# A long convolution by four transform stages and two MLPs on one core: each half's fourth stage follows its third, and the spectral product is stored channel by channel

## The chip, the cores and the metric

One core of a Trainium2 chip (trn2) runs the whole program. The metric is the device time of one execution in microseconds.

## The reference

For 12480 positions and 128 channels, `x` and `v` are given. A small network makes a filter of the same length for each channel, `h = relu(pos_emb @ w1) @ w2`, times a decay over positions. Then

```python
u = x * v
Uf, Hf = rfft(u, n=2 * S), rfft(h_filt, n=2 * S)
y = irfft(Uf * Hf, n=2 * S)[:S]
x1 = x * y
x2 = square(relu(x1 @ moe_w_in)) @ moe_w_out
g = x2 @ moe2_w_in
out = (g * sigmoid(1.702 * g)) @ moe2_w_out
```

with a hidden width of 2048 in both MLPs. All inputs are float32.

## The kernel before

Positions are an array of A = 104 rows by B = 120 columns. The transform of twice that length is four rounds of matrix products with constant tables.

- The filter network comes first (lines 703 to 724).
- Stage 1 (`step1`, line 731) transforms over the 104 rows, for 64 channels (a half, `h`) of the filter H and then of u. Its results are copied to Z, 124 partitions.
- Stage 2 (`step2`, line 780) transforms over the columns in NG = 26 groups of four frequencies. A group is 4 products of 256 columns. ACT copies the filter's half of the spectrum from PSUM (`copy_h`, line 604), VectorE multiplies (`products`, lines 663 to 673) into `prod_s` and `prod_x`, and GpSimd combines these into the real and imaginary product P with one subtraction and one addition (`combine_p`, lines 332 to 337; `combine`, line 519). Group 25 is combined by VectorE (line 679). `prod_s` and `prod_x` have two buffers each. P is laid out [120 partitions][frequency 104][real, imaginary][channel 64].
- Stage 3 (`step3`, line 745) transforms back over the columns, in 16 groups of four channels. P is the stationary operand, `P[h][:, :, r, 4 * k + e]`, 104 columns with a step of 128 elements. ACT copies two edges and the imaginary part (lines 615 to 624), and VectorE makes a difference and a sum of it for Y (lines 681 to 689), iterating channel, real/imaginary, column.
- Stage 4 (`step4`, line 397) transforms back over the rows and brings both halves' channels to positions. It comes once, after both halves' stages 1 to 3: 15 groups plus a single column group, each with both halves, with tables in a ring `t4` of four. 12 groups and the single column are done before the MLPs, 3 groups (LATE) inside the first MLP tile at positions 2, 4 and 6 of its order (`LATE_AT`). ACT and VectorE copy 64 partitions at a time to XT (lines 379 to 395), GpSimd multiplies x and y to a tile (`stage`, line 917).
- The MLPs (`mlps`, line 816) run over 30 tiles of 416 positions, each product as three products of rounded parts (lines 1005 to 1010). Weights are loaded raw, rounded by ACT (`make_hi`) and split by GpSimd (`split_low`, two operations for each of four weights).

So the halves run 1, 2, 3, 1, 2, 3, 4, MLP. Stages share four PSUM slots of two banks; a slot's user waits on `free[q]`. SP's queue issues nearly all loads in the order written out at lines 444 to 492 and waits in that order. In stage 2 it refills a ring of four spectrum table buffers `f_ring` (240 KB each) as TensorE leaves them. Ahead of that in the first half it issues `load_u(1, 0)` and `load_u(1, 1)` (four loads of 390 KB); in the second half, four t4 tables (338 KB each) and the last column's. `load_u(1, i)` brings x and v of 8 channels, which GpSimd multiplies and folds (`make_u`, lines 495 to 505, one product and two sums); for the second half this starts right behind the first half's combinations. Small products on constants (`spare_products`) fill TensorE's waits between stages.

Of the kernel before, what the change touches and what calls it, by code (L numbers as in the profile page):

```python
# [5 lines left out]
S = 12480  # L6
A, B = 104, 120
L = 2 * S
# [27 lines left out]
LATE = 3  # L36
EARLY = [*range(JG - LATE), JG]
LATE_AT = {2: JG - 3, 4: JG - 2, 6: JG - 1}
# [3 lines left out]
Y_HALF = B * D  # L42
HR = 2 * Y_HALF
BIG = HR + 2 * HC * BR
U_ZONE = HC * BR
U_SLACK = 3 * 2 * FG * 2 * HC


def constant_tables(w1, w2):
# [14 lines left out]
    t4.append(2 * np.pi * np.outer(f + 0.5, (a - A // 2) * B + B) / L)  # L64
# [16 lines left out]
def s4_units(g):  # L81

    return g + 1 + (g >= JG - LATE)


def tile_rows(t):

    g = t // 2
    if t % 2 == 0:
        return [TB * g + i for i in range(TB)]  # L90
    if g == JG - 1:
        return [B - 1, *range(B - 1 - LOW + 1, B - 1 - LOW + TB)]
    return [B - 1 - TB * (g + 1) + i for i in range(TB)]


TILE_ORDER = [b for t in range(NT) for b in tile_rows(t)]
# [8 lines left out]
def by_tile(z):  # L105

    return z.reshape(A, B, D)[:, TILE_ORDER].transpose(2, 1, 0).reshape(D, S)


def from_tiles(z):  # L110

    out = np.empty((A, B, D), z.dtype)
    out[:, TILE_ORDER] = z.reshape(D, B, A).transpose(2, 1, 0)
    return out.reshape(S, D)


def build(nc, x_ch, v_ch, x_t, pos_emb, w_in1, w_out1, w_in2, w_out2,
# [10 lines left out]
    with ExitStack() as ctx:  # L128
# [9 lines left out]
        with ExitStack() as shared:  # L138
            mlp = mlp_buffers(lambda name, shape, dt=F32: sb(name, shape, dt, shared), F32R)
        conv = conv_buffers(sb)  # L140
        XT = conv["big"][:, HR:HR + S].rearrange("p (t n) -> p t n", n=TN)

        first = {name: sem(name) for name in (
            "s4_full", "xt_low", "xt_high", "x_t_in0", "x_t_in1", "staged", "x1_hi", "x1_lo")}
        w_hi_made = [sem(f"w_hi_made{m}") for m in range(4)]
        w_split = [sem(f"w_split{m}") for m in range(4)]
        weights = (w_in1, w_out1, w_in2, w_out2), w_in_dma, mlp["w_hi"], mlp["w_lo"], w_hi_made, w_split

        block = ctx.enter_context(nc.Block())
        late = convolution(nc, block, sem, ALU, ACT, ds, F32, ps, conv, mlp, XT, weights, first,  # L150
                           x_ch, v_ch, x_t, pe_d, net, fwd1, fwd2_d, inv3, inv4, identity)
        mlps(nc, block, sem, ALU, ACT, ds, F32, XT, ps, mlp, weights, first, late, x_t, out)


def conv_buffers(sb):

    return {
        "big": sb("big", [128, BIG]),
        "u_zone": sb("u_zone", [128, U_ZONE]),
        "t3": sb("t3", [B, 184]),  # L160
        "t1": sb("t1", [A, 2, 2 * A]),
        "f_ring": sb("f_ring", [128, RING, FG, B]),
    }


def mlp_buffers(sb, F32R):
# [8 lines left out]
    def skip_to(where):  # L175
        assert where >= at[0], (where, at[0])
        if where > at[0]:
# [3 lines left out]
           "in_hi": [None] * 2, "in_lo": [None] * 2, "x_tile": [None] * 2}  # L181
    pair = [128, 2, TN]

    out["w_lo"][2] = put("w_lo2", [128, DFF], F32R)
    out["w_lo"][3] = put("w_lo3", [128, DFF], F32R)
    out["relu"] = put("relu", pair)
    out["act_f"] = [put(f"act_f{s}", pair) for s in range(NS)]
    out["act_hi"] = [put(f"act_hi{s}", pair, F32R) for s in range(4)]
    out["yT"] = put("yT", [128, TN])
    assert at[0] <= Y_HALF - LATE * TB * 2 * D  # L190
    skip_to(Y_HALF)
    out["w_hi"][2] = put("w_hi2", [128, DFF], F32R)
    out["w_hi"][3] = put("w_hi3", [128, DFF], F32R)
    out["act_hi"] += [put(f"act_hi{s}", pair, F32R) for s in range(4, NB)]
    out["act_lo"] = [put(f"act_lo{s}", pair, F32R) for s in range(NB)]
    out["in_hi"][1] = put("in_hi1", [128, TN], F32R)
    out["in_lo"][1] = put("in_lo1", [128, TN], F32R)
    assert at[0] <= 2 * Y_HALF - LATE * TB * 2 * D
    skip_to(HR + S)
    out["in_hi"][0] = put("in_hi0", [128, TN], F32R)  # L200
    out["in_lo"][0] = put("in_lo0", [128, TN], F32R)
    assert at[0] == HR + A * 2 * HC + 2 * TN - (A * 2 * HC - S)
    out["w_hi"][0] = put("w_hi0", [128, DFF], F32R)
    out["x_tile"][0] = put("x_tile0", [128, TN])
    skip_to(BIG)
    out["w_lo"][0] = put("w_lo0", [128, DFF], F32R)
    out["w_lo"][1] = put("w_lo1", [128, DFF], F32R)
    skip_to(BIG + U_ZONE - (RING * TB * TAB + TAB))
    out["t4"] = put("t4", [128, RING, TB, TAB])
# [880 lines left out]
```

## Time and profile before

| | us |
|---|---|
| median of 3 runs | 1504.84 (1504.59 to 1507.27) |
| the profiled execution | 1502.83 |
| its span | 1501.0 |
| TensorE busy in it | 1477.3 |
| ScalarE (ACT) busy | 999.2 |
| VectorE (DVE) busy | 914.5 |
| GpSimd (POOL) busy | 197.3 |

The profile is of one execution, and its durations are compared with its own time. PEld is the load of the stationary operand, which overlaps products. Products are pipelined, so the recorded duration of one is longer than the pace; the pace comes from a stage's time divided by its instructions. Of a product in full float32 the trace has two instructions.

### The profile page before, as it was taken

The numbers are of one execution on the slowest core, as the hardware profiler recorded it, in microseconds if no ns is written. First come the engines' busy times: TensorE is split into PE (matmuls) and PEld (weight loads), VectorE is DVE, ScalarE is ACT, GpSimd is POOL, SyncE is SP. The second block draws the span as 40 slices with busy tenths as digits, with TensorE's granted clock in tenths as the row PEclk, the third lists the DMA queues.
The fourth block names the chain that finished last, engine by engine and source line by source line (L and its number), as shares of the span: only waits on it lengthen the run. The fifth ranks groups of instructions, "written<-read, shape, count | busy, mean of one in ns | idle before, by whom it ended". The sixth has DMA issues, their size and how long they took to land.

```text
span 1501.0 us, 22451 instructions
## 1 busy us (share of the span) xinstructions
PE 1477.3 (98%) x7970; PEld 1434.4 (96%) x7970; DVE 914.5 (61%) x1198; ACT 999.2 (67%) x1404; POOL 197.3 (13%) x192
## 2 busy tenths in 40 slices
PE   8999999999999999999999999999999999999998
PEld 6987998899989999999999999999999999999997
DVE  3668576663556666666666666666666566666664
ACT  6643254323577777777777777777777777777775
POOL 5418802602300000000000000000000000000000
PEclk9999999999999999999999999999999999999999
DMA  8223503405100000000000000000000000000000
GB/s 224 74 78 110 154 1 93 124 1 158 46 1 12 12 11 11 11 11 11 11 11 11 11 12 19 15 11 11 11 11 11 11 11 11 12 11 11 6 6 12
DMA packets 28344, 52.06 MB, mean 35 GB/s; under 512 B 3060, under 2 KB 22140, under 8 KB 28052
## 3 DMA queue, kind: packets, MB, share of 16 engines
q1 hardware_dynamic: 27768, 51.02, 11.5%
q10 hardware_dynamic: 540, 0.55, 0.1%
q8 instruction: 23, 0.38, 0.1%
q14 instruction: 13, 0.11, 0.0%
HBM read 45.17 MB, written 6.39 MB: 34 GB/s over the span
## 4 chain that ended last, share of the span: by engine, by line
PE 96%; DVE 1%; DMA 1%; ACT 1%; issue 1%; SPq 0%; ACTq 0%
PE ps L1008 24%; PE ps L1010 24%; PE ps L1009 24%; PE ps L751 6%; PE ps L741 6%; PE ps L786 5%; PE ps L408 3%; PE ps L722 2%; DMA f_ring<-in_fwd 1%; PE ps L715 1%; DVE act_lo L996 1%; PE ps L707 0%; PE ps L729 0%; ACT act_f L951 0%; DVE act_hi L994 0%
## 5 line engine op out<-in xcount | busy, mean ns | idle before, releaser
L996 DVE TENSOR_TENSOR act_lo<-act_f,act_hi 128x832 fp32r<-128x832 f32 x480 | 489.1, 1029 | 126.8 <-ACT act_hi L954 118.5
L1008 PE MATMUL ps<-in_hi,w_hi 128*128 128x416 f32 x960 | 338.4, 353 | 6.4 <-DVE in_lo L968 2.6
L1008 PE MATMUL ps<-act_hi,w_hi 128*128 128x416 f32 x960 | 339.0, 353 | 0.9 <-DVE act_lo L996 0.9
L1009 PE MATMUL ps<-act_lo,w_hi 128*128 128x416 f32 x960 | 337.5, 352 | 0.0
L1010 PE MATMUL ps<-act_hi,w_lo 128*128 128x416 f32 x960 | 336.7, 351 | 0.0
L1010 PE MATMUL ps<-in_hi,w_lo 128*128 128x416 f32 x960 | 336.3, 350 | 0.0
L1009 PE MATMUL ps<-in_lo,w_hi 128*128 128x416 f32 x960 | 336.2, 350 | 0.0
L994 DVE CAST act_hi<-act_f 128x832 fp32r<-128x832 f32 x240 | 143.7, 599 | 296.9 <-ACT act_f L949 296.9
L944 ACT ACTIVATE relu<-ps 128x832 f32<-128x832 f32 x240 | 208.3, 868 | 131.7 <-PE ps L1010 127.4
L951 ACT ACTIVATE act_f<-ps 128x832 f32<-128x832 f32 x240 | 207.0, 862 | 107.5 <-PE ps L1010 107.3
L949 ACT ACTIVATE act_f<-relu 128x832 f32<-128x832 f32 x240 | 215.9, 900 | 22.1 <-DVE act_lo L996 0.4
L954 ACT ACTIVATE act_hi<-ps 128x832 fp32r<-128x832 f32 x240 | 206.0, 858 | 0.0
L1008 PEld LDWEIGHTS ps<-in_hi,w_hi 128*128 128x128 f32 x960 | 180.2, 188 | 10.0 <-issue 5.1
L1008 PEld LDWEIGHTS ps<-act_hi,w_hi 128*128 128x128 f32 x960 | 179.7, 187 | 3.9 <-DVE act_lo L996 2.0
L1010 PEld LDWEIGHTS ps<-act_hi,w_lo 128*128 128x128 f32 x960 | 180.9, 188 | 2.6
L1009 PEld LDWEIGHTS ps<-in_lo,w_hi 128*128 128x128 f32 x960 | 180.1, 188 | 2.6
L1010 PEld LDWEIGHTS ps<-in_hi,w_lo 128*128 128x128 f32 x960 | 180.3, 188 | 2.2
L1009 PEld LDWEIGHTS ps<-act_lo,w_hi 128*128 128x128 f32 x960 | 180.2, 188 | 1.7
L751 PEld LDWEIGHTS ps<-t,big 120*104 120x104 f32 x512 | 91.9, 273 | 4.2 <-issue 4.2
L751 PE MATMUL ps<-t,big 120*104 120x120 f32 x512 | 92.2, 344 | 3.7 <-issue 3.7
L786 PE MATMUL ps<-big,f_ring 124*120 (+1 forms) x416 | 90.7, 380 | 4.0 <-DMA f_ring<-in_fwd 3.4
L786 PEld LDWEIGHTS ps<-big,f_ring 124*120 124x120 f32 x416 | 75.8, 183 | 18.7 <-issue 4.2
(79 smaller groups left out, 1118.9 us busy)
## 6 DMA issues: line engine op xcount, KB each, us to landing
f_ring<-in_fwd SPq DMA_DIRECT2D x52, 240.0 KB, 2.6
big<-in_x_by_channel SPq DMA_DIRECT2D x16, 390.0 KB
big<-in_v_by_channel SPq DMA_DIRECT2D x16, 390.0 KB
out<-yT SPq DMA_DIRECT2D x30, 208.0 KB, 1.9
t<-in_inv SPq DMA_DIRECT2D x15, 338.0 KB
big<-in_pos_emb SPq DMA_DIRECT2D x40, 78.0 KB
x_tile<-in_x_by_tile SPq DMA_DIRECT2D x15, 208.0 KB, 2.6
t<-in_x_by_tile SPq DMA_DIRECT2D x15, 208.0 KB, 2.5
```

The lines of the kernel that those rows point to most:

```text
L741: mm = nc.tensor.matmul(slot[q][0:BR, e // 2, at:at + 2 * A], data, t1[:, 1 if k < N1 // 2 else 0, :], start=True, stop=True)
L751: mm = nc.tensor.matmul(slot[q][0:A, e // 2, at:at + W3], P[h][:, :, r, 4 * k + e], t3[:, r * (LOW + 1):r * (LOW + 1) + W3], start=True, s ...
L786: mm = nc.tensor.matmul(flat[s][0:B, j * 2 * D:(j + 1) * 2 * D], f_ring[0:BR, s, j, :], Z[h][:, :, ds((k * FG + j) * 2 * HC, 2 * HC)], sta ...
L944: nc.scalar.activation(relu[:, :, :], slot[s], ACT.Relu).then_inc(relu_done, 1)
L949: nc.scalar.activation(act_f[s][:, :, :], relu[:, :, :], ACT.Square).then_inc(act_done[0], 1)
L951: nc.scalar.activation(act_f[s][:, :, :], slot[s], ACT.Gelu_apprx_sigmoid)
L954: nc.scalar.activation(act_hi[p % NB][:, :, :], slot[s], ACT.Gelu_apprx_sigmoid)\
L994: nc.vector.tensor_copy(hi[:, :, :], f[:, :, :]).then_inc(hi_done, 1)
L996: nc.vector.tensor_tensor(lo[:, :, :], f[:, :, :], hi[:, :, :].bitcast(F32), ALU.subtract)\
L1008: nc.tensor.matmul(to, w_hi[w][:, cols], hi, start=first, stop=False)
L1009: nc.tensor.matmul(to, w_hi[w][:, cols], lo, start=False, stop=False)
L1010: return nc.tensor.matmul(to, w_lo[w][:, cols], hi, start=False, stop=last)
```

## The change

It does three things.

1. The fourth stage of a half follows its third: 1, 2, 3, 4, 1, 2, 3, 4, MLP. A group now has one half in one bank, 128 partitions by 416 positions, and ACT alone copies it (`keep_xy`) to X[h]. The first half has 15 groups, the second 10 ahead of the MLPs and 5 (LATE) inside the first tile, at positions 2, 4, 6, 16 and 17, copied by VectorE. Each half's t4 tables are loaded. The two halves' rows are brought together by DMAs (`load_xy`) into `xy_tile`, from which GpSimd multiplies.
2. Memory is laid out anew, and loads move in SP's queue with it. In the first half, no load of x and v is issued ahead of stage 2's tables; all eight pieces come after the combination. In both halves the first four refills of `f_ring` are ahead of what follows. GpSimd waits for VectorE's last combination before it folds.
3. P is laid out [120 partitions][channel 64][real, imaginary][frequency 104]. The combination iterates channel and then frequency, and VectorE's third-stage operations iterate column and then channel.

```diff
-LATE = 3
-LATE_AT = {2: JG - 3, 4: JG - 2, 6: JG - 1}
+LATE = 5
+LATE_AT = {2: JG - 5, 4: JG - 4, 6: JG - 3, 16: JG - 2, 17: JG - 1}
...
-    P = [carve(big, B, (h + 1) * Y_HALF, A, 2, HC)[0] for h in range(2)]
+    P = [carve(big, B, at, HC, 2, A)[0] for at in P_AT]
...
         rows = ds(k * FG, FG)
-        s, x = prod_s[h][:, half], prod_x[h][:, half]
-        tensor_tensor(P[h][:, rows, 0, :], s[:, :, 0, :], s[:, :, 1, :], ALU.subtract)
-        tensor_tensor(P[h][:, rows, 1, :], x[:, :, 0, :], x[:, :, 1, :], ALU.add).then_inc(p_done[half], 1)
+        to = P[h][:, :, :, rows].rearrange("p c r f -> p r c f")
+        s, x = (prod[h][:, half].rearrange("p f r c -> p r c f") for prod in (prod_s, prod_x))
+        tensor_tensor(to[:, 0], s[:, 0], s[:, 1], ALU.subtract)
+        tensor_tensor(to[:, 1], x[:, 0], x[:, 1], ALU.add).then_inc(p_done[half], 1)
...
-                    mm = nc.tensor.matmul(slot[q][0:A, e // 2, at:at + W3], P[h][:, :, r, 4 * k + e],
+                    mm = nc.tensor.matmul(slot[q][0:A, e // 2, at:at + W3], P[h][:, 4 * k + e, r, :],
...
-                low, high = (Y[h][:, 0:LOW - 1, :, m, c4].rearrange("p j r c -> p c r j") for m in (h, 1 - h))
-                re2 = re.rearrange("p c (r j) -> p c r j", r=2)[:, :, :, 1:LOW]
-                im2 = im_copy[h][:, k % 2].rearrange("p c (r j) -> p c r j", r=2)[:, :, :, 0:LOW - 1]
+                low, high = (Y[h][:, 0:LOW - 1, :, m, c4].rearrange("p j r c -> p r j c") for m in (h, 1 - h))
+                re2 = re.rearrange("p c (r j) -> p r j c", r=2)[:, :, 1:LOW, :]
+                im2 = im_copy[h][:, k % 2].rearrange("p c (r j) -> p r j c", r=2)[:, :, 0:LOW - 1, :]
...
+    def keep_xy(copy, h, g, q):
+
+        to, made, last = X[h][:, g], ps[:, 2 * q, 0:TN], ps[:, 2 * q + 1, TN - A:TN]
+        if g < JG - 1:
+            return copy(to, made)
...
+    def load_xy(sp, t):
+
+        n, g = t % 2, t // 2
+        sp.dma_start(mlp["x_tile"][n][:, :], x_t[:, t * TN:(t + 1) * TN]).then_inc(x_t_in[n], 16)
+        for h in range(2):
+            rows = slice((t + h) % 2 * HC, ((t + h) % 2 + 1) * HC)
+            sp.dma_start(mlp["xy_tile"][n][h * HC:(h + 1) * HC, :], X[h][rows, g]).then_inc(x_t_in[n], 16)
...
         for h in range(2):
-            if h == 0:
-
-                stage_done(sp, "s1", 0)
-                load_u(1, 0)
-                load_u(1, 1)
-            else:
+            for s in range(RING):
+                load_f(h, 1, s)
+            if h == 1:
 
                 stage_done(sp, "s1", 1)
                 for g in range(RING):
-                    load_t4(g)
-                sp.dma_start(t4_last[0:A, :], inv4[:, JG * TB * TAB:]).then_inc(t4_last_in, 16)
-            with sp.Fori(1, F_FULL) as i:
+                    load_t4(sp, 1, g)
+                sp.dma_start(t4_last[1], inv4[:, JG * TB * TAB:]).then_inc(t4_last_in, 16)
+            with sp.Fori(2, F_FULL) as i:
...
             if h == 0:
+                for g in range(RING):
+                    load_t4(sp, 0, g)
+                for i in range(PIECES):
+                    if i >= X_SLOTS:
+
+                        sp.wait_ge(u_folded, PIECES + i - X_SLOTS + 1)
+                    load_u(1, i)
+                    if i == X_SLOTS - 1:
+                        sp.dma_start(t4_last[0], inv4[:, JG * TB * TAB:]).then_inc(t4_last_in, 16)
+                load_t4_behind(0, range(RING, JG))
+
+                stage_done(sp, "s4", 0)
                 for s in range(RING):
                     sp.dma_start(f_ring[:, s], fwd2_d[:, s * FG:(s + 1) * FG, :]).then_inc(ld_f[s], 16)
...
+        for m in range(3):
+            load_w(m)
+        stage_done(sp, "s3", 1)
+        load_w(3)
+        load_t4_behind(1, range(RING, RING + 2))
+
+        s4_done(sp, 0)
+        sp.wait_ge(free[0], used["s4", 1][0] + 1)
+        load_xy(sp, 0)
+        load_t4_behind(1, range(RING + 2, JG - 1))
...
             if h == 0:
+
+                p_made(pool, 0)
+                stage_done(pool, "s2", 0)
+                nc.gpsimd.memset(U[1][:, :, LOW:ODD], 0.0)
                 for i in range(PIECES):
                     make_u(1, i)
...
+            for k, spare in ((N3 - 4, 1), (N3 - 3, 2), (N3 - 2, 2)):
+                q = k % RING
+                pe.wait_ge(free[q], used["s3", h][q] + k // RING + 1)
+                spare_products(q, spare)
+            y_made(pe, h)
+            for g in range(JG - h * LATE):
+                q = g % RING
+                pe.wait_ge(free[q], used["s4", h][q] + g // RING)
+                step4(pe, h, g, q, full[q])
```

`load_t4_behind` waits for TensorE to leave a group's table buffer before it loads the next into it. ACT rounds the four weights at groups 0, 2, 5 and 8 of the second half's fourth stage.

## Rows read from the trace of the kernel before

**Rows 1.** The profile's part 1: busy time (share of the span) and instructions of each engine.
```profile
PE 1477.3 (98%) x7970; PEld 1434.4 (96%) x7970; DVE 914.5 (61%) x1198; ACT 999.2 (67%) x1404; POOL 197.3 (13%) x192
```

**Rows 2.** Busy time by stage: window, its length, then PE, PEld, DVE, ACT, POOL busy (x instructions), clock, DMA.
```profile
98.10:145.20 47.10, 45.25 (x209) 38.09 (x210) 33.42 (x75) 14.63 (x25) 33.62 (x48) 1.00 0.53 148
...
150.99:197.08 46.09, 46.09 (x256) 46.09 (x257) 26.71 (x30) 10.39 (x45) 33.01 (x22) 0.97 0.41 126
342.20:386.19 43.99, 43.99 (x392) 43.81 (x392) 14.39 (x25) 16.18 (x27) 14.81 (x7) 1.00 0.55 159
```

**Rows 3.** Groups by line and form, TensorE's loads: busy us, mean ns, idle before.
```profile
L751 PEld LDWEIGHTS ps<-t,big 120*104 120x104 f32 x512 | 91.9, 273 | 4.2 <-issue 4.2
L786 PEld LDWEIGHTS ps<-big,f_ring 124*120 124x120 f32 x416 | 75.8, 183 | 18.7 <-issue 4.2 <-DVE big L318 1.1
L408 PEld LDWEIGHTS ps<-t,big 104*128 104x128 f32 x480 | 54.1, 192 | 1.6 <-issue 1.5
...
L722 PEld LDWEIGHTS ps<-big 128*104 128x104 f32 x120 | 21.1, 176 | 7.5 <-ACT big L557 0.3 <-issue 0.2
```

**Rows 4.** TensorE in order of time: start us, us, what, idle before it.
```profile
107.09 38.24 PE L786 MATMUL ps<-big,f_ring 124*120 x176 [1.84 <-DMA f_ring<-in_fwd]
...
150.99 46.26 PE L751 MATMUL ps<-t,big 120*104 120x120 f32 x256 [3.21 <-issue]
...
243.58 7.14 PE L786 MATMUL ps<-big,f_ring 124*120 124x256 f32 x32 [0.29 <-DVE big L318]
252.28 38.22 PE L786 MATMUL ps<-big,f_ring 124*120 x176 [1.56 <-DMA f_ring<-in_fwd]
...
293.40 45.98 PE L751 MATMUL ps<-t,big 120*104 120x120 f32 x256 [0.46 <-issue]
...
342.20 43.10 PE L408 MATMUL ps<-t,big 104*128 104x104 f32 x384 [1.29 <-DVE big L689]
```

**Rows 5.** Groups by line and form, VectorE: third stage, products, first stage's copies.
```profile
L318 DVE COPY big<-ps 64x832 f32<-64x832 f32 x32 | 32.5, 1017 | 23.9 <-PE ps L741 23.9
...
L670 DVE TENSOR_TENSOR u_zone<-ps,u_zone 120x512 f32<-120x512 f32 x26 | 18.0, 691 | 14.0 <-ACT u_zone L609 14.0
...
L688 DVE TENSOR_TENSOR big<-ps,u_zone 104x472 f32<-104x472 f32 x16 | 15.4, 963 | 20.4 <-ACT u_zone L624 20.4
```

**Rows 6.** GpSimd in order of time, combinations of the second stage.
```profile
102.30 0.72 POOL L336 TENSOR_TENSOR big<-big 120x256 f32 x1 [47.88 <-DVE big L672]
...
142.36 0.73 POOL L336 TENSOR_TENSOR big<-big 120x256 f32 x1 [0.31 <-DVE big L672]
143.05 0.73 POOL L337 TENSOR_TENSOR big<-big 120x256 f32 x1
144.09 0.72 POOL L336 TENSOR_TENSOR big<-big 120x256 f32 x1 [0.31 <-DVE big L672]
```

**Rows 7.** Groups by line and form, GpSimd: product of x and v, fold, weight split.
```profile
L501 POOL TENSOR_TENSOR big<-big 104x960 f32<-104x960 f32 x16 | 35.7, 2229 | 19.2 <-DMA big<-in_v_by_channel 19.2
...
L503 POOL TENSOR_TENSOR u_zone<-big 104x480 f32<-104x480 f32 x16 | 19.3, 1208 | 1.3
...
L511 POOL TENSOR_TENSOR w_lo<-u_zone,w_hi 128x1024 fp32r<-128x1024 f32 x4 | 9.3, 2352 | 64.9 <-ACT w_hi L571 64.9
```

**Rows 8.** VectorE's last combination beside GpSimd's folding (order of time), and alone (groups).
```profile
147.07 2.20 POOL L501 TENSOR_TENSOR big<-big 104x960 f32<-104x960 f32 x1
...
147.37 2.18 DVE L336 TENSOR_TENSOR big<-big 120x256 f32<-120x256 f32 x1
...
L336 DVE TENSOR_TENSOR big<-u_zone 120x256 f32<-120x256 f32 x1 | 0.4, 424 | 0.0
```

**Rows 9.** The window after TensorE's longest idle time, columns as in rows 2.
```profile
151.00:152.00 1.00, 1.00 (x5) 1.00 (x6) 0.00 (x0) 0.00 (x0) 1.00 (x2) 0.50 0.08 13
```

**Rows 10.** SP's queue in order of time at the second half's tables, and the loads' sizes.
```profile
242.35 1.57 SPq L432 DMA_DIRECT2D t<-in_inv  x4
...
t<-in_inv SPq DMA_DIRECT2D x15, 338.0 KB
```

More of the change, by code:

```diff
@@ L163, in conv_buffers, with raw_weights @@
     }
+def raw_weights(sb):
+    w_raw, end = [None] * 4, 0
+    for m, at in ((3, X_SIZE + DFF), (0, Z_AT[1][0]), (1, Z_AT[1][0] + 2 * DFF), (2, Z_AT[1][0] + 4 * DFF + 3 * TN)):
+        sb(f"below_w_raw{m}", at - end)
+        w_raw[m] = sb(f"w_raw{m}", DFF)[:, :]
+        end = at + DFF
+    return w_raw
 def mlp_buffers(sb, F32R):
@@ L214, in mlp_buffers @@
-    out["x_tile"][1] = out["t4"][:, 3, 0:2, :].rearrange("p i w -> p (i w)")
+    out["stage"] = put("stage", [128, TN])
+    out["w_lo"][2] = put("w_lo2", [128, DFF], F32R)
+    for n in range(2):
+        out["x_tile"][n] = put(f"x_tile{n}", [128, TN])
+        out["xy_tile"][n] = put(f"xy_tile{n}", [128, TN])
+    skip_to(Y_AT[1])
+    out["act_hi"] = [put(f"act_hi{s}", pair, F32R) for s in range(NB)]
+    out["act_lo"] = [put(f"act_lo{s}", pair, F32R) for s in range(NB)]
+    assert at[0] <= Y_AT[1] + (JG - LATE) * TB * 2 * D
@@ L215, in mlp_buffers, with convolution @@
+    skip_to(Y_AT[1] + Y_SIZE)
+    out["relu"] = put("relu", pair)
+    out["yT"] = put("yT", [128, TN])
+    skip_to(IM_AT[1])
+    out["act_f"] = [put("act_f0", pair)]
+    skip_to(BIG)
+    out["act_f"] += [put(f"act_f{s}", pair) for s in range(1, NS)]
     return out
-def convolution(nc, block, sem, ALU, ACT, ds, F32, ps, buf, mlp, XT, weights, first,
+def convolution(nc, block, sem, ALU, ACT, ds, F32, ps, buf, mlp, X, weights, first,
                 x_ch, v_ch, x_t, pe_d, net, fwd1, fwd2_d, inv3, inv4, identity):
@@ L301, in convolution @@
     for h in range(2):
-        for name, groups in (("s1", N1), ("s2", NG), ("s3", N3)):
+        for name, groups in (("s1", N1), ("s2", NG), ("s3", N3), ("s4", JG - h * LATE)):
             used[name, h] = list(n)
@@ L308, in convolution @@
     P_USES = [len(range(s, NG, 2)) for s in range(2)]
+    T4_USES = [len(range(s, JG, RING)) for s in range(RING)]
     def step1_channels(k, h):
@@ L412, in _, with s4_done @@
+    def load_xy(sp, t):
[4 more added lines that the diff above has]
+            sp.dma_start(mlp["xy_tile"][n][h * HC:(h + 1) * HC, :], X[h][rows, g]).then_inc(x_t_in[n], 16)
+    def s4_done(eng, h):
+        for q in range(RING):
+            eng.wait_ge(free[q], used["s4 end", h][q])
     @block.sync
@@ L895, in _ @@
     def _(sp):
[L896 to L900 removed]
+        for q in range(RING):
+            banks_free(sp, q)
+        load_xy(sp, 1)
+        sp.wait_ge(s4_late, 1)
+        load_t4(sp, 1, JG - 1)
         sp.wait_ge(staged, 1)
[L902 removed]
+        load_xy(sp, 2)
         for r in range(NT):
@@ L1045, in part @@
                     if found is None:
-                        before = max(n for n in range(len(EARLY)) if n % RING == p % NS)
-                        pe.wait_ge(xt_low, min(before + 1, JG - LATE))
-                        pe.wait_ge(xt_high, before + 1)
+                        banks_free(pe, p % NS)
                     else:
```

305 lines of the change are left out of this document (126 added, 179 removed).

## The prediction

> **What bounds the kernel now.** I read the engine shares first, then the busy time by stage, then TensorE's loads by form, then the order of time where stages meet. TensorE is busy 98% of the span [rows 1], so only its speed in a stage, or its idle time between stages, can move the end. The stages of one half of the channels are: the second (208 TensorE instructions, with GpSimd at 33.62 of 47.10 us), the third (256 in 46.09 us) and the fourth (392 in 43.99 us, for both halves) [rows 2]. A product in full precision is recorded as two instructions, so the numbers per instruction below are halves of a product.
>
> The third stage stands out. Its 256 instructions take 46.26 us, 181 ns each, though each streams 120 columns only. The second stage streams 256 columns in 38.24/176 = 217 ns, 0.85 ns a column. The loads say why: a load of 104 columns takes 273 ns where the operand is read with a step of 512 bytes, and 176 to 192 ns where 104, 120 or 128 columns lie side by side [rows 3]. In the windows of rows 2, loading is busy for the whole of the third stage and for 38.09 of 47.10 us of the second.
>
> **The change part by part.**
>
> *The third stage.* With side-by-side columns the load no longer sets the pace. Streaming would be 120 x 0.85 = 102 ns; the fourth stage, 104 columns streamed and 128 loaded side by side, has 43.99/392 = 112 ns. I take 104 ns, bounds 102 and 112: 256 x 0.104 = 26.6 us for a half, against 46.26 and 45.98 us [rows 4]. VectorE must keep up: 16 groups of two operations, 963 ns each on the record. Today they read runs and write with a 1 KB step, where a 512-element operation with unstrided writes takes 691 ns, so the step costs about 0.6 ns an element; the new order writes runs of 16 bytes, as a copy of 832 elements in 1017 ns does at full pace, but its SBUF input gets a 480-byte step [rows 5]. Bounds 0.65 and 0.96 us for one, 1.3 to 1.9 us for a group against TensorE's 1.66; recorded operations overlap a little, so I take 1.69. Third stage: 27.0 us a half, together **-38.2 us**.
>
> *The combination on GpSimd.* This pays for it. Today each group has a pair of subtractions and additions of 120x256, 0.73 us each and 1.42 us together, and then 0.31 us of waiting: GpSimd has 18% to spare in a period of 1.73 us [rows 6]. Afterwards both inputs are read with a step of 512 bytes and the output is written in runs of four. No GpSimd row with such a step exists. From contiguous rows, 2229 ns for 960 elements and 1208 for 480, an operation is 0.19 us plus 2.13 ns an element [rows 7]. The lower bound is no change. For the middle I take the two strided prices of other engines: TensorE's load, (273-176)/104 = 0.9 ns a column [rows 3], and VectorE's 0.6 ns an element [rows 5]. Two inputs make 1.2 to 1.8 ns more, so one operation is 1.04 to 1.19 us, a pair 2.0 to 2.3. I take 2.15 us, as these are the nearest strided accesses. The upper bound is two strided accesses in turn at their whole recorded cost, VectorE's 963/472 = 2.0 ns or the load's 273/104 = 2.6 ns, 1.2 to 1.5 us for one operation.
>
> The Trainium skill's GPSIMD Engine Reference, "Performance pitfalls for Q7 kernels", says that a GpSimd kernel reading SBUF with a step over 8 bytes pays about 2.9 cycles an element instead of 1.9, half as much again. No row here shows it. By it on the whole element cost, one operation would be 1.0 us and the pair 1.95, five microseconds less per half than my term; if its extra cycle, at the page's 1.2 GHz, is paid for each input, the pair is 2.25.
>
> At 2.15 us GpSimd sets the pace of the second stage. Its first pair starts 4.2 us after the stage's first product (102.30 [rows 6], where the stage's window begins at 98.10 [rows 2]). 25 groups then take 53.8 us. The last group is combined by VectorE, which has two inputs in SBUF: beside a GpSimd operation this took 2178 ns, alone 424 [rows 8], so I add 1.0 us. The third stage then begins 59.0 us after the second. Today it is 150.99-98.10 = 52.9 us and 293.40-243.58 = 49.8 us [rows 4]. **+6.1 and +9.2 us**. In the first half this already includes the removal of two waits: 3.21 us before 150.99, since the new wait keeps GpSimd's folding off VectorE's last combination, and 1.84 us before 107.09, where the spectrum table stood behind four loads of x and v [rows 4, 8]. After those 3.21 us of idle time the granted clock was 0.50, 1.2 of 2.4 GHz, in the window from 151 us [rows 9]; today's load-bound products hardly feel that, streaming-bound ones would, and a slow GpSimd leaves a like wait. **+1.0 us** for both halves.
>
> *The fourth stage cut in two.* The same 488 instructions remain; 244 now run behind the first third stage, 160 before the MLP and 84 inside it. ACT alone copies them, one 128-row copy per group. In the old stage ACT and VectorE together were busy 30.6 of 43.99 us [rows 2], so that is hidden. What is new is a second passage from third to fourth: 293.40+45.98 = 339.38 to 342.20 [rows 4], **+2.8 us**.
>
> *Loads moved past each other.* All eight pieces of x and v for the second half now leave behind four t4 loads, and t4 group 4 leaves behind the eighth piece, which waits until five pieces are folded. A piece costs GpSimd 2.23+2x1.21 = 4.65 us [rows 7]. The first needs 1.4 MB of tables and 0.8 MB of its own: some 12 us, from the 1.68 MB that took 252.28-242.35 = 9.9 us [rows 4, 10]. So five pieces are done at 35 us behind the combination, and t4 group 4 lands about 6 to 7 us later, 42. TensorE wants it at 27.0+2.8+4x1.8 = 37. **+4 us**, bounds 0 and 6. The folding itself ends at 12+37 = 49 us, long before its reader. In the second half the t4 tables now leave after 4 spectrum loads, some 7.5 us into the stage. The same 9.9 us put the next spectrum table at 17.4, wanted at 8x1.73 = 13.9 with today's pace, 17.2 with GpSimd's: nothing beside 2.15 us, but 3.5 instead of 1.56 us if GpSimd is not the bound.
>
> *The MLP's start.* Weights have 18 us of fourth stage instead of 44, and GpSimd needs 2.35 us per split, eight of them [rows 7]. The first two and the first product of x and y fit; the last two end some 4 us into the first tile, as now, and are wanted two tiles later. Five late groups of the fourth stage are spread over the first tile instead of three double ones. The rest of the MLP keeps its instructions; the xy tiles come by DMAs that SP issues a tile ahead. 0, bounds -1.5 and +2.
>
> **Sum:** -38.2+15.3+1.0+2.8+4 = -15.1. The profiled execution took 1502.8 us; 1487.7 by its own time. It lies 2.0 us under the median of the runs, 1504.84, so I forecast 1489.
>
> **The rivals.**
>
> *GpSimd stays hidden* (pair at most 1.7 us). For it: it has 0.31 us to spare, and its 2.13 ns an element is slow enough to hide a slower fetch. Then the second stages take 52.9-1.84-2.75 = 48.3 and 49.8+1.9 = 51.7 us, -2.7 instead of +15.3; with -38.2+1+2.8+4 that is -33: **1472**, and 1468 without the t4 wait.
>
> *GpSimd takes away more than the third stage gives.* This one ends slower. Place: the same pairs. If GpSimd serves its two strided reads in turn, an operation is 1.4 us, between 1.2 and 1.5 of the upper bound, and the pair 2.8: 4.2+70+1 = 75 us per second stage, +22+25 = +47, -38+47+3 for the slow clock after longer idle+2.8+4 = +19: **1523**. It decides from where the second stages grow by 30 us together, a pair of 2.45 us. Against it: no strided row adds over 0.9 ns an element, and this needs 1.3 for each input.
>
> Read as 2.9 cycles for each input in turn, the Trainium skill's figure (the same page and section) would lead here.
>
> *The third stage doesn't speed up*, since VectorE's new order is slower than the old one, 1.3 us and more an operation, or since the load's 273 ns do not come from the step. Third stage 41 us a half gives only 10 back: 1500 with a hidden GpSimd, **1518** with a slow one. The side-by-side loads of rows 3 speak against the second reason.
>
> **How the numbers follow.** Forecast 0.43, hidden 0.30, GpSimd too slow 0.17, third stage not faster 0.06, something else 0.04, shared out. The range 1466 to 1512 takes in the first two with their bounds and the near part of the others; the forecast's own range is 1478 to 1502. A measurement can tell 0.2%, 3 us. Faster 0.78, same 0.03, slower 0.19.
>
> **What would show it.** Loads of the third stage near 176 ns instead of 273, and its 256 instructions in 26 to 28 us. GpSimd's pair: at 1.42 us the first rival holds, at 2.0 to 2.3 my sum, over 2.45 the second. If it is slow, GpSimd shows no waiting in the second stage while TensorE waits about 0.4 us a group. No 3.21 us wait ahead of the first third stage by contention with folding. A wait for a t4 table near the fifth group of the first fourth stage. I am wrong if GpSimd's pair is unchanged, or if VectorE rather than TensorE paces the third stage.

## The result and the profile after

The changed kernel takes **1517.05 us** (median of 8 runs, 1514.91 to 1526.48); the kernel before, run beside it, 1504.71. The ratio is **1.0096, 95% interval 1.0079 to 1.0113**: slower by 1%, outside the predicted range and on the other side of no change. The profiled execution took 1517.49 us, its span is 1515.7. Where the times of one kernel fall into separate groups, ratios and intervals are those of its faster group (here one run of the kernel before, 1542.66 us, is outside).

The page of the changed kernel, engines and granted clock in 40 slices of 37.9 us:

```profile
PE 1479.1 (98%) x7980; PEld 1430.2 (94%) x7980; DVE 901.2 (59%) x1173; ACT 998.0 (66%) x1401; POOL 230.8 (15%) x193
...
PEclk9999857999999999999999999999999999999999
```

TensorE is 98% busy, as before [rows 1], and busy for 1.8 us longer, although its third stage was to lose some 38 us of busy time. The clock line says where to look: a dip to 0.5 in the slice from 189 us. The windows by stage of the changed kernel follow (bounds, length, busy time and instructions of PE, PEld, DVE, ACT, POOL, then granted clock, DMA share, GB/s):

```profile
98.05:147.50 49.45, 48.32 (x208) 36.89 (x208) 31.12 (x69) 14.05 (x24) 45.27 (x44) 1.00 0.41 110
155.39:184.32 28.93, 28.93 (x257) 28.93 (x258) 23.88 (x27) 10.88 (x45) 16.33 (x12) 0.91 0.78 200
189.50:241.65 52.15, 52.15 (x245) 52.15 (x245) 0.00 (x0) 7.08 (x14) 15.31 (x11) 0.50 0.36 96
241.65:288.89 47.24, 47.24 (x258) 47.04 (x258) 31.76 (x45) 28.42 (x50) 0.00 (x0) 0.95 0.07 22
290.37:343.85 53.48, 49.18 (x209) 39.48 (x209) 31.11 (x69) 14.06 (x24) 45.26 (x44) 0.94 0.48 129
351.70:379.77 28.07, 28.07 (x256) 28.07 (x257) 23.81 (x28) 10.90 (x45) 0.00 (x0) 0.94 0.33 113
384.75:403.24 18.49, 18.07 (x160) 17.93 (x161) 1.65 (x1) 10.09 (x13) 11.74 (x7) 1.00 0.68 180
```

In order: second, third and fourth stage of half 1, first, second, third and fourth of half 2. Against [rows 2], the third stage fell from 46.09 to 28.93 us. The fourth stage of the first half took 52.15 us for 244 instructions, **at a granted clock of 0.50** throughout: 214 ns an instruction, where the last row has 18.49/160 = 116 ns. A busy engine at 1.2 of its 2.4 GHz looks like any busy engine in the shares.

TensorE in order of time (start, duration, line, tiles, count; in brackets the idle time before and what ended it):

```profile
151.65 1.18 PE L742 MATMUL ps<-t 120*120 120x180 f32 x6 [1.20 <-DVE big L689]
155.39 29.09 PE L764 MATMUL ps<-t,big 120*104 120x120 f32 x256 [2.56 <-issue]
...
185.69 0.87 PE L742 MATMUL ps<-t 120*120 120x180 f32 x4 [0.90 <-DVE big L706]
187.44 0.95 PE L742 MATMUL ps<-t 120*120 120x180 f32 x4 [0.88 <-DVE big L706]
189.50 7.13 PE L392 MATMUL ps<-big 104*128 104x104 f32 x32 [1.10 <-DVE big L706]
...
308.38 33.31 PE L799 MATMUL ps<-big,f_ring 124*120 x136 [3.97 <-DMA f_ring<-in_fwd]
...
351.70 28.23 PE L764 MATMUL ps<-t,big 120*104 120x120 f32 x256 [2.05 <-issue]
...
380.82 0.87 PE L742 MATMUL ps<-t 120*120 120x180 f32 x4 [0.58 <-DVE big L706]
382.60 0.87 PE L742 MATMUL ps<-t 120*120 120x180 f32 x4 [0.91 <-DVE big L706]
384.75 10.94 PE L392 MATMUL ps<-big 104*128 104x104 f32 x96 [1.28 <-DVE big L706]
...
414.23 0.71 PE L1030 MATMUL ps<-in_hi,w_hi 128*128 128x416 f32 x1 [3.80 <-DVE big L400]
```

"Passage" below means the short stretch between a third and a fourth stage, with TensorE's waits for VectorE and the products on constants (spares, L742). The slow stage begins behind a passage in which TensorE waited 0.90, 0.88 and 1.10 us, with ten spare instructions among the waits. The passage of the second half has 0.58, 0.91 and 1.28 us and keeps its clock. Two-microsecond windows of the same kernel show the fall and the return:

```profile
186.00:188.00 2.00, 1.12 (x8) 0.84 (x6) 2.00 (x3) 0.22 (x1) 2.00 (x2) 1.00 0.53 108
188.00:190.00 2.00, 0.90 (x5) 0.56 (x4) 1.13 (x2) 0.00 (x0) 1.92 (x2) 0.52 0.75 230
...
244.00:246.00 2.00, 2.00 (x7) 1.90 (x7) 0.00 (x0) 1.24 (x2) 0.00 (x0) 0.50 0.99 345
246.00:248.00 2.00, 2.00 (x13) 2.00 (x12) 1.10 (x2) 0.52 (x2) 0.00 (x0) 0.97 0.08 30
```

So the clock was down from about 188 us, before the last of the three waits ended, and it came back only 4 us into the next stage. The groups of the combination (L343; L344 is its addition) and of the third stage:

```profile
L764 PEld LDWEIGHTS ps<-t,big 120*104 120x104 f32 x512 | 57.0, 181 | 5.3 <-issue 5.3
L343 POOL TENSOR_TENSOR big<-big 120x256 f32 x48 | 54.3, 1132 | 140.8 <-DVE big L689 140.8
...
L687 DVE TENSOR_TENSOR big<-ps,big 120x512 f32<-120x512 f32 x52 | 36.0, 692 | 45.4 <-POOL big L344 32.7 <-ACT big L630 12.7
L705 DVE TENSOR_TENSOR big<-ps,big 104x472 f32<-104x472 f32 x32 | 31.7, 991 | 9.5 <-ACT big L645 9.5
```

A load of the third stage takes 181 instead of 273 ns [rows 3]; a GpSimd operation 1132 instead of 730 ns [rows 6], and VectorE now waits 32.7 us for it (L687).

Starts of the stages on TensorE, before and after, give the whole account (us; the second stage begins at 98.1 in both):

| stretch | before | after | difference |
|---|---|---|---|
| second stage to third, half 1 | 52.89 | 57.34 | +4.45 |
| third stage, half 1 | 46.26 | 28.93 | -17.33 |
| passage and fourth stage, half 1 | none | 5.18 + 52.15 | +57.33 |
| first stage of half 2, to its second | 46.33 | 48.72 | +2.39 |
| second stage to third, half 2 | 49.82 | 61.33 | +11.51 |
| third stage, half 2 | 45.98 | 28.07 | -17.91 |
| passage to the last fourth stage | 2.82 | 4.98 | +2.16 |
| that fourth stage, to the MLPs | 45.00 | 18.49 | -26.51 |
| MLPs | 1113.8 | 1112.5 | -1.3 |
| sum | | | +14.8 |

This is the difference of the two spans, 14.7 us, but for rounding and the 0.05 us by which the second stage begins earlier in the changed kernel.

### The profile page after: what moved, and what is told of

It is laid out like the page before. It is cut to its first block, busy times and chain, and to the rows that moved or that the text cites. A ratio compares the mean times of both kernels' runs of the same rounds, so it can differ in the third digit from the quotient of the medians.

```text
span 1515.7 us, 22527 instructions
## 1 busy us (share of the span) xinstructions
PE 1479.1 (98%) x7980; PEld 1430.2 (94%) x7980; DVE 901.2 (59%) x1173; ACT 998.0 (66%) x1401; POOL 230.8 (15%) x193
## 4 chain that ended last, share of the span: by engine, by line
PE 86%; DVE 5%; POOL 4%; issue 2%; DMA 1%; ACT 1%; SPq 0%; POOLq 0%; ACTq 0%; DVEq 0%
PE ps L1030 24%; PE ps L1031 24%; PE ps L1032 24%; PE ps L754 6%; PE ps L392 5%; POOL big L343 3%; DVE big L705 2%; DVE big L706 2%; PE ps L735 2%; POOL big L344 2%; PE ps L799 1%; PE ps L728 1%; PE ps L764 1%; DMA f_ring<-in_fwd 1%; DVE act_lo L1018 0%
## 5 line engine op out<-in xcount | busy, mean ns | idle before, releaser
L943 POOL TENSOR_TENSOR stage<-xy_tile,x_tile 128x416 f32<-128x416 f32 x29 | 32.2, 1112 | 971.6 <-DVE in_lo L990 971.6
L799 PE MATMUL ps<-big,f_ring 124*120 (+1 forms) x416 | 97.5, 391 | 6.0 <-DMA f_ring<-in_fwd 4.0
L754 PE MATMUL ps<-t,big 104*124 104x208 f32 x512 | 92.7, 345 | 0.3 <-DVE big L666 0.3
```

What stands on the lines that cost most here:

```text
L754: mm = nc.tensor.matmul(slot[q][0:BR, e // 2, at:at + 2 * A], data, t1[:, 1 if k < N1 // 2 else 0, :], start=True, stop=True)
L799: mm = nc.tensor.matmul(flat[s][0:B, j * 2 * D:(j + 1) * 2 * D], f_ring[0:BR, s, j, :], Z[h][:, :, ds((k * FG + j) * 2 * HC, 2 * HC)], sta ...
```

## The experiments

**Theory**: the waits in the passage from third to fourth stage drop the clock, and the fourth stage's products run at half clock until the stage ends. **Rivals**: something else in the new kernel slows its first fourth stage (its layout, its tables, GpSimd beside it), or the reorganisation itself costs the time and the clock is only a part.

**Spares in the passage.** The wait becomes work on constants; nothing else changes.

```diff
-(N3 - 4, 1), (N3 - 3, 2), (N3 - 2, 2)
+(N3 - 4, 4), (N3 - 3, 5), (N3 - 2, 5)
```

> The changed kernel with more products on constants in TensorE's three waits between third and fourth stage (4, 5, 5 instead of 1, 2, 2). Theory A: the waits of 0.90, 0.88 and 1.10 us there let the clock fall, and it then stays at 0.50 for the whole fourth stage of the first half. Filled, the clock stays 1.00, the 244 instructions take 27.4 us instead of 52.2, the next first stage 45.3 instead of 47.3: 1517 - 27 = 1490 us. Rival B: the fourth stage in its new form (one half, tables in the spectrum ring) runs at 0.50 by itself; then nothing changes, 1517 us.

Measured: two groups of runs, six of 1489.6 to 1496.1 us (ratio 0.9925, 0.9909 to 0.9941) and five of 1512.4 to 1516.1. The first group is near the 1490 us expected. The profiled execution is of the second. Its TensorE in order of time, then its windows:

```profile
182.56 4.95 PE L742 MATMUL ps<-t 120*120 120x180 f32 x28
187.82 3.79 PE L392 MATMUL ps<-big 104*128 104x104 f32 x32 [0.31 <-DVE big L706]
...
198.25 5.74 PE L392 MATMUL ps<-big 104*128 104x104 f32 x32 [3.06 <-DMA big<-in_inv]
203.78 7.03 PE L392 MATMUL ps<-f_ring,big 104*128 104x104 f32 x32
```

```profile
188.00:198.00 10.00, 7.18 (x64) 7.01 (x63) 0.00 (x0) 2.02 (x4) 9.77 (x8) 1.00 0.75 204
...
204.00:234.00 30.00, 30.00 (x142) 30.00 (x142) 0.00 (x0) 4.54 (x9) 0.36 (x1) 0.50 0.25 70
```

With the passage filled, 32 instructions take 3.79 us instead of 7.13: the fall at the stage's start is gone, and with it the rival of a slow layout or slow tables. What is left is the wait for t4 group 4 that the prediction named: 3.06 us at the fifth group (16 instructions each), and behind it the clock falls after all. At half clock the tables had been in time, which hid this wait. No run of the faster group was profiled, so that their clock held is read from their times alone.

**The reorganisation alone**, with P, combination and third stage as before:

```diff
-    P = [carve(big, B, at, HC, 2, A)[0] for at in P_AT]
+    P = [carve(big, B, at, A, 2, HC)[0] for at in P_AT]
```

> The changed kernel with P, the combination and both third-stage parts as before: the fourth stage behind the third, alone. Theory A: the third stage takes 46 us a half again, VectorE isn't behind TensorE at its end, the waits ahead of the fourth stage are short and the clock stays 1.00 in it; pairs on GpSimd 1.42 us, second stages 48 and 51 us. Time 1501 to 1507 us, like before. Rival B: the fourth stage of the first half is at 0.50 here too, 52 us: 1526 to 1532 us.

Measured: median 1509.3; five runs of 10 lie at 1502.8 to 1503.9, the others at 1514.7 to 1538.1. The ratio, 1.0017 (0.9987 to 1.0047), is of the seven up to 1516.1. The profiled one is of the first: its fourth stage of half 1 takes 27.3 us (194.64 to 221.94) at clock 1.00. So moving the fourth stage costs nothing on the whole when the clock holds, and the longer times show that the new order can lose time without the new layout. No execution of those was profiled, so which wait did it is open.

**The combination reads contiguously and writes with a step.** The same values to the same places, frequency ahead of channel: inputs in runs, output in steps of 832 bytes.

```diff
-        to = P[h][:, :, :, rows].rearrange("p c r f -> p r c f")
-        s, x = (prod[h][:, half].rearrange("p f r c -> p r c f") for prod in (prod_s, prod_x))
+        to = P[h][:, :, :, rows].rearrange("p c r f -> p r f c")
+        s, x = (prod[h][:, half].rearrange("p f r c -> p r f c") for prod in (prod_s, prod_x))
```

> The changed kernel, its combination iterating frequency and then channel: GpSimd reads runs of 64 elements and writes with a step of 832 bytes. Theory C: the 1.13 us of a GpSimd operation come from its strided reads; back to 0.73 here, pair 1.42, second stages 9 and 10 us shorter, 1517 - 19 = 1498 us, or 1471 if the clock also holds ahead of the first fourth stage. Rival D: a strided write costs GpSimd as much as strided reads; the pair stays at 2.2 us, 1517 us.

The group of GpSimd's subtraction in that kernel, then its TensorE in order of time:

```profile
L343 POOL TENSOR_TENSOR big<-big 120x256 f32 x48 | 35.4, 738 | 152.3 <-DVE big L689 152.3
```

```profile
145.51 26.46 PE L764 MATMUL ps<-t,big 120*104 120x120 f32 x256 [0.73 <-issue]
...
173.32 0.87 PE L742 MATMUL ps<-t 120*120 120x180 f32 x4 [1.03 <-DVE big L706]
175.06 0.87 PE L742 MATMUL ps<-t 120*120 120x180 f32 x4 [0.87 <-DVE big L706]
177.12 7.13 PE L392 MATMUL ps<-big 104*128 104x104 f32 x32 [1.19 <-DVE big L706]
```

738 ns, as before: the price of the new combination is all in its strided reads, and this step of 832 bytes between written elements costs GpSimd nothing. The third stage starts 9.9 us earlier than in the changed kernel, takes 26.46 us and has no slow start. Yet the kernel took 1507.78 us, ratio 1.0027 (1.0016 to 1.0038), a miss: both fourth stages ran at half clock, the second one too (160 instructions in 33.9 us, behind waits of 0.75, 0.90 and 1.20 us), where the changed kernel's had held. The gain of the second stage was given back by the clock.

**The fall by itself, in the kernel before**, without the spares ahead of its fourth stage:

```diff
-            spare_products(q, spare)
         y_made(pe, 1)
```

> The kernel of before without the five products on constants ahead of its fourth stage (the waits stay). Theory A: the waits let the clock fall, and in the fourth stage it doesn't come back: 44 us become 80 or more, 1505 + 36 = 1541 us or more. Rival E: it comes back within some 6 us, as behind the other falls of the changed kernel (161, 315, 355 and 420 us): 1508 us. Rival F: the clock doesn't fall at all: 1505 us.

TensorE in order of time, then a window of that stage:

```profile
342.34 81.88 PE L408 MATMUL ps<-t,big 104*128 104x104 f32 x384 [2.82 <-DVE big L689]
```

```profile
342.34:400.00 57.66, 57.66 (x272) 57.66 (x273) 10.01 (x17) 10.42 (x18) 10.18 (x5) 0.50 0.36 104
```

Measured: 1544.18, ratio 1.0265 (1.0245 to 1.0285). **One idle time of 2.82 us costs 39 us**: 384 instructions take 81.88 us instead of 43.10 [rows 4], with neither the new order nor the new layout. In the kernel before the spares hold this off, though not always: 8 of the 25 runs of it beside these four kernels took 1541.5 to 1543.9 us, close to the time of this one. None of those was profiled.

**Loads in another order.** The third kernel above with the filled passage; half 2's t4 tables behind its spectrum tables; t4 groups 4 to 7 of half 1 ahead of the eighth piece of x and v, and the fourth MLP weight behind t4 group 7.

```diff
             for s in range(NG % RING):
                 load_f(h, F_FULL, s)
+            if h == 1:
+                for g in range(RING):
+                    load_t4(sp, 1, g)
...
                 for i in range(PIECES):
+                    if i == PIECES - 1:
+                        load_t4_behind(0, range(RING, 2 * RING))
```

> The kernel of f3_rows_in with the products on constants of f1_spares and three loads moved: the second half's t4 tables behind all spectrum tables, t4 groups 4 to 7 of the first half ahead of the eighth piece of x and v, the fourth weight behind t4 group 7. Theory A: with the waits gone the clock stays at 1.00 in both fourth stages. 1507.5 - 24.8 (first fourth stage 27.4) - 15.7 (second 18.2) - 2.3 (first stage behind it) - 5 (the wait of 3.67 us in the second half's second stage and its slow clock) = 1460 us. Rival: one half's fourth stage falls to 0.50 by itself sooner or later, or table loads cannot keep up at 1.8 us a group: 1480 to 1507 us.

Measured: 1483.58, ratio 0.9855 (0.9839 to 0.9872). The 4 us wait for a spectrum table is gone. But t4 waits of 2.68 us (half 1) and 1.84 us (half 2) were left, and behind each the clock fell: almost 24 us more than the 1460 expected.

**VectorE's imaginary input side by side.** In addition, ACT writes `im_copy` with the channel inside, so that VectorE's operations in the third stage read it in runs of four, as they write.

```diff
-    im_copy = [carve(big, A, at, 2, 4, W3)[0] for at in IM_AT]
+    im_copy = [carve(big, A, at, 2, W3, 4)[0] for at in IM_AT]
```

> The kernel of g1_order, and ACT stores the copy of the imaginary part column by column, channel inside, so that VectorE reads it in runs of four and only PSUM with a step. Theory G: VectorE's 0.98 us an operation in the third stage come from the strided read in SBUF, as 0.96 us before came from the strided write; 0.65 to 0.70 here, TensorE waits less ahead of each fourth stage: 3 to 5 us less than g1_order. Rival H: the 16-byte runs or the step in PSUM cost the same; 0.98 us, no change.

The group in the kernel before this step, and in this one:

```profile
L709 DVE TENSOR_TENSOR big<-ps,big 104x472 f32<-104x472 f32 x32 | 32.5, 1016 | 5.4 <-ACT big L649 5.4
```

```profile
L709 DVE TENSOR_TENSOR big<-ps,big 104x472 f32<-104x472 f32 x32 | 20.8, 650 | 18.5 <-ACT big L649 18.5
```

1016 to 650 ns, with the input from PSUM as strided as before: it is the SBUF step that VectorE pays for. The time is 1479.99, ratio 0.983 (0.9814 to 0.9847). The runs of this kernel (1477.8 to 1484.8) and of the one before this step (1480.8 to 1484.9) overlap, so the 3 to 5 us expected are neither shown nor refuted: t4 waits (3.99 and 2.19 us in the profiled run) still drop the clock.

**Weights prepared earlier.** In addition, the first two MLP weights are rounded and split during the last third stage.

```diff
-    HI_AT, FIRST_HI_AT = {0: 0, 2: 1, 5: 2, 8: 3}, 7
+    HI_AT, FIRST_HI_AT = {0: 2, 8: 3}, 7
```

> The kernel of g2_im, and the first two weights are rounded and split during the second half's third stage, the third at the start of its fourth. Theory I: in the first MLP tile VectorE's two-input operations took 1.4 to 3.1 us beside GpSimd's splits instead of 0.6 to 1.0, and TensorE waited 3.8 us for VectorE's late copy; with one split left beside it that wait is gone: 3 to 5 us less than g2_im. Rival J: ACT is the bound in that tile, or what is saved is waited for later: within 1 us of g2_im.

Measured: 1465.86, 1478.42, 1484.69 and 1485.14 us, ratio 0.9854 (0.9829 to 0.9878). The 3.80 us wait in the first MLP tile is 0.22 us here, but it had already shrunk to 0.47 us and to none in the profiled runs of the two kernels before this step, whose last fourth stage ran partly at half clock; that more time for the weights did this was not tested. The profiled run, the fastest, held 1.00 through its first fourth stage and lost it in the second behind a wait of 2.77 us. The median says nothing on this step, for which 3 to 5 us were expected; the spread is as large as the cost of a fall.

**The same order with the changed kernel's strided combination**, against the one with new order above:

> The kernel of g1_order, but with the changed kernel's combination (GpSimd reads with a step). What the change would take if no wait let the clock fall in a fourth stage: 1517 - 27 (clock in and behind the first fourth stage) - 6 (the wait of 3.97 us in the second half and its slow clock) = 1484 us, and 22 to 26 us more than g1_order, which prices the strided reads: two second stages 9 to 11 us longer and the clock behind them. Rival: the passage from second to third stage is the cause of the low clock here; then first fourth stage at 0.50 again, 1510 us.

Measured: 1505.71, ratio 1.0002 (0.9993 to 1.0012), 22 us over its neighbour: the diff is the combination's two lines alone. I had expected 1484 us, 22 to 26 more than the neighbour, for which 1460 stood; the difference was right, the 1460 wasn't. In the profiled runs both kernels lose their clock in both fourth stages. TensorE at the end of the second half's, in this kernel:

```profile
384.20 3.81 PE L392 MATMUL ps<-big 104*128 104x104 f32 x32 [2.08 <-DMA big<-in_inv]
390.72 7.13 PE L392 MATMUL ps<-big 104*128 104x104 f32 x32 [2.72 <-DMA big<-in_inv]
```

Behind the wait of 2.08 us the clock stayed at 1.00, where 1.84 us had been enough in the neighbour; behind 2.72 us it fell.

**Tables that are never late.** The pieces 6 to 8 of x and v leave behind all t4 tables of half 1, and half 2 has six t4 buffers instead of four (two in the spectrum ring, free by then), filled ahead of its stage. The fourth MLP weight is again loaded ahead of the late t4 groups. The rest is as in the kernel with the weights prepared earlier.

```diff
-                    if i == PIECES - 1:
-                        load_t4_behind(0, range(RING, 2 * RING))
+                    if i == PIECES - 3:
+                        load_t4_behind(0, range(RING, JG))
...
+        load_t4(sp, 1, 4)
+        load_t4(sp, 1, 5)
         for m in range(3):
             load_w(m)
```

> The kernel of g3_weights with the t4 waits inside the fourth stages taken away: pieces 6 to 8 of x and v behind all t4 tables of the first half, and six table buffers instead of four for the second half's early groups (two in the spectrum ring). Theory A: no wait is left in a fourth stage, the clock stays at 1.00 through both, 27.4 and 17.9 us, and the runs no longer spread over 20 us: 1465.9 (the fastest g3_weights) - 5.5 (its waits) - 3.6 (two groups at 0.50) = 1457 us. Rival: the clock falls in a fourth stage without a wait too; 1465 to 1485 us, spread as before.

TensorE in order of time, then windows of the two fourth stages:

```profile
145.88 26.46 PE L779 MATMUL ps<-t,big 120*104 120x120 f32 x256 [0.73 <-issue]
...
176.45 3.71 PE L402 MATMUL ps<-big 104*128 104x104 f32 x32
...
189.69 2.00 PE L402 MATMUL ps<-f_ring,big 104*128 104x104 f32 x16 [0.58 <-DMA f_ring<-in_inv]
```

```profile
174.00:202.00 28.00, 27.42 (x240) 27.27 (x239) 0.31 (x1) 6.58 (x13) 6.39 (x5) 1.00 0.55 150
326.00:346.00 20.00, 20.00 (x172) 20.00 (x171) 1.88 (x4) 7.93 (x13) 5.73 (x3) 1.00 0.62 164
```

Measured: **1455.36 us (1455.08 to 1456.27), ratio 0.9674 (0.9661 to 0.9687)**, as expected within 2 us, and the runs now lie within 0.1% of each other. The longest t4 wait left is 0.58 us. This beats both kernels.

**The change's two terms in the kernel whose clock holds**: first the strided combination (the two lines above, back), then the layout of before.

> The kernel of k1_ring6 with the changed kernel's combination. It prices GpSimd's strided reads where no fourth stage loses its clock: two second stages 9.0 us longer (57.3 against 48.3 to the third stage) and 2.6 us each for the slow clock at the third stage's start, so 23 us more than k1_ring6, 1480 us. Rival: part of that is hidden by what else ends late; under 15 us more.

> The kernel of k1_ring6 with P as before (frequency outside, channel inside), its combination and the stationary operand read with a step of 512 bytes. It prices the layout alone where no fourth stage loses its clock. Theory: the third stages take 46.0 instead of 26.5 us each and the pair 1.42 instead of 1.48: 1455 + 39 = 1494 us, so that the changed kernel's layout, with the slow combination (1478 us in k2_ring6_slow), is worth 16 us and the forecast's sum of -38 and +23 was right. Rival: the old layout hides other work that k1_ring6 pays for; under 1485 us.

The third stages of the two kernels, in order of time:

```profile
155.51 29.03 PE L779 MATMUL ps<-t,big 120*104 120x120 f32 x256 [2.54 <-issue]
```

```profile
146.09 45.98 PE L778 MATMUL ps<-t,big 120*104 120x120 f32 x256 [0.46 <-issue]
```

1477.64 (ratio 0.9822, 0.9808 to 0.9835) and 1493.81 (0.9933, 0.9918 to 0.9948), both as expected within 3 us. The layout with strided reads is worth 1493.81 - 1477.64 = **16.2 us**; with contiguous reads 38.45 us; the strided reads cost 22.3 us. Of these, 18.0 us are the two second stages (57.3 instead of 48.3 us to the third stage) and most of the rest the slow clock at the start of both third stages. The kernel with the old layout was run beside other runs of the kernel before (median 1504.01 us) than the other two (1504.26).

**Spares in the kernel before** (1, 3 and 6 instead of 1, 2 and 2):

> The kernel of before with 1, 3 and 6 instead of 1, 2 and 2 products on constants ahead of its fourth stage. Theory A: its own rare slow times (1542 to 1544 us in 10 of 56 runs) are the same fall of the clock ahead of the fourth stage; none here, all runs at 1503 to 1506 us. Rival: they come from somewhere else and are still there now and then.

Measured: 1503.58 (1502.55 to 1503.94, 11 runs), ratio 0.9996 (0.9986 to 1.0005). No gain in the usual run, and none of its 11 runs was at 1543, where 3 of 15 runs of the kernel before beside it were. In all its comparisons 13 of 71 runs of the kernel before were there; at that rate 11 clean runs come about once in ten, so this supports the reading and doesn't prove it.

## Why the prediction was wrong

*What bounds the kernel, and the rows read first*: right. Only TensorE's pace in a stage or its idle time moved the end; the pace moved in two stages.

*Third stage, 27.0 us a half*: 28.93 and 28.07 us here, 26.46 wherever it starts at full clock; loads 169 ns there. The source of the 273 ns was the step. VectorE's operation lay just over the upper of my bounds, 0.65 and 0.96 us (991 ns; pairs overlap to 1.79 us a group). My reading of the old step's price, 0.6 ns an element, was low: 963/472 - 691/512 is 0.7. So VectorE fell behind TensorE's 1.66 us a group, and TensorE waited for it in the passage.

*The combination, 2.15 us a pair*: right. Operations start every 1.04 us, so that a pair takes 2.07 us. GpSimd in the second stage of the changed kernel, in order of time:

```profile
120.97 1.14 POOL L343 TENSOR_TENSOR big<-big 120x256 f32 x1
122.01 1.14 POOL L344 TENSOR_TENSOR big<-big 120x256 f32 x1
```

Second to third stage took 57.3 and 61.3 us against 59.0 each, together +16.0 for my +15.3; the pair of kernels whose clock holds in both fourth stages prices the strided reads at 22.3, as their contiguous version has a shorter second stage than the kernel before. The step added 1132 - 738 = 394 ns to 256 elements, 1.54 ns each, 0.77 for each of two inputs. The Trainium skill (GPSIMD Engine Reference, "Performance pitfalls for Q7 kernels") has 2.9 cycles instead of 1.9 for strided reads. Its one extra cycle, paid for each input at the page's 1.2 GHz, is an estimate of 0.83 ns; paid once, it would be half of what was measured. The whole operation grew by 1132/738 = 1.53, which the page's ratio gives too. The page's rule is on reads; that this written step was free is what the third experiment shows. The folding is off VectorE's last combination, as I had expected (1.02 and 0.67 us instead of 2.18 and 1.41). The wait ahead of the third stage remained all the same, 2.56 us behind two more of 0.89 and 1.20 us, now at GpSimd's pace.

*The spectrum tables of half 2, "nothing beside 2.15 us"*: wrong. TensorE waited 3.97 us for one at 308.38. SP issued four spectrum loads from 292.4, then four t4 tables and the last column's to 300.1, and only then the next spectrum load. I had put its landing at 17.4 us of the stage, and it was used at 18.0 (308.38 - 290.37). It was wanted at 14.0, as with today's pace (13.9 in my text), not at the 17.2 that I took from GpSimd's: TensorE ran its first 64 instructions in 14.04 us, ahead of GpSimd, while buffers were free.

***+1.0* us for the slow clock: the step that failed.** I had seen the low clock of [rows 9] and wrote that streaming-bound products would feel it, and then charged 1 us for the two third stages, as if it always came back in a few microseconds. There it does: 155 to 161 us is at 0.52 and the rest of the stage at 1.00, though even that cost more than my term, since the two stages took 2.6 and 1.8 us longer than one at full clock (26.30 us to its end). I did not ask what the fourth stage does at half clock, nor what state the passage hands over to it. It stayed at half clock for all 52.15 us, where 27.30 would have done (the second experiment): **+24.9 us**, and 2.2 more in the next stage (47.24 against 45.03 there). The spares experiment removes the fall at the stage's start, the fourth one makes it in the kernel before. Without these 27.1 us the span is 1488.6, against 1501.0 - 15.1 = 1485.9 by my sum. The agreement is partly of errors that cancel: the passages cost 7.3 us and not 2.8, the third stages 57.0 and not 54.0, while the tables' wait of 4 us did not show. (The sum itself gives 1489.7 as median; I wrote 1489.)

*The new passage, +2.8 us*: 5.2 and 5.0 us. I copied the old passage and not VectorE's lag, and took its waits at their own length. The larger price was the clock behind them.

*t4 group 4, +4 us*: not seen in the changed kernel, since the slow stage wanted its tables later; 3.06 us as soon as the stage started at full clock. The reckoning was right and its price too low once more: five of 11 runs took some 20 us longer than the others, and the one of them that was profiled lost its clock behind this wait.

*The MLP's start, 0*: -1.3 us in the account, by errors that cancel. A wait of 3.80 us is new, and the clock is at 0.50 behind it from 414 to 420 us. GpSimd's splits ended 7.1 us into the first tile (410.3 - 403.2), where I had put 4. Against it stand 12 instructions less at 112 ns, 1.3 us, and something that I had not foreseen: a tile of the MLPs takes 36.23 us instead of 36.37 (the distance between GpSimd's products for successive tiles), about 4 us over the 29 that follow. No run shows which part of the change did this. VectorE beside GpSimd's weight splits, then alone, in the changed kernel:

```profile
408.17 3.07 DVE L1018 TENSOR_TENSOR act_lo<-act_f,act_hi 128x832 fp32r<-128x832 f32 x1
...
412.64 1.02 DVE L1018 TENSOR_TENSOR act_lo<-act_f,act_hi 128x832 fp32r<-128x832 f32 x1
```

In the kernels whose last fourth stage held its clock and whose weights were split late, this wait was 3.80, 3.59 and 3.76 us (the changed kernel, the first and the second experiment); with the weights split earlier and the same clock it was 0.21 us (the kernel whose tables are never late). The Trainium skill (SBUF — State Buffer, "Who interferes with whom") says that VectorE's second port pair is GpSimd's too and locked by either; 3.07 against 1.02 us for an operation with two SBUF inputs agrees.

*The rivals*: "GpSimd stays hidden" and "the third stage doesn't speed up" fell by their groups. The slower rival had the right sign for the wrong reason: its pair of 2.8 us was 2.07. My list had no case in which the clock ends the account, though a row showed it falling.

What stays open: what exactly separates the passage of half 1 (0.90, 0.88, 1.10 us, clock lost) from that of half 2 (0.58, 0.91, 1.28 us, held), why the third experiment lost its clock behind 0.75, 0.90 and 1.20 us, why a wait of 2.08 us held where one of 1.84 us did not, and why equal kernels differ from run to run. The runs show which waits went before a fall, not a rule for it.

## What to carry to other kernels

Ask of every wait on TensorE what stage stands behind it. Here a wait of 1.8 to 4 us ahead of or inside the fourth stage mostly cost not itself but the rest of the stage at half clock, and in two kernels three waits of about 1 us did so too. A stage at half clock still reads as 100% busy, so look at the granted clock by stage before the shares. Where GpSimd must either read or write with a step, try the step on its write: here that was free, and on its two reads it cost half the operation again. Judge a moved stage by the order in which its queue delivers tables, and keep the tables ahead of it, before judging its arithmetic.

## What was not expected of the hardware

- The clock that fell ahead of a fourth stage did not return within 52 us (changed kernel) or 81.9 us (fourth experiment), at 100% busy; it returned 4 us into the first stage of half 2, and within 6 us in the third stages.
- GpSimd's 256-element operation: 729 ns when it reads and writes in runs, 738 ns when it writes in steps of 832 bytes; 1132 ns with reads in steps of 512 bytes.
- VectorE's 472-element operation: 650 ns when its SBUF input and output lie in runs of four, with the PSUM input still read with a step; 991 to 1016 ns with a 480-byte step in the SBUF input too.
